# Attention and two mixture layers on one core: two operand loads before two stores, one cast after the exponentials, one pair's values before queries

## The reference

```python
scores = where(block_i >= block_j, q @ k.T / sqrt(64), -1e9)   # blocks of 64
x = softmax(scores) @ v                       # 4 x 8 heads -> (2304, 512)
p = probs / probs.sum(-1)
x = sum(p[:, e] * (relu(x @ w1[e]) @ w2[e]) for e in range(4))  # 512 -> 1024 -> 512
h = x @ w_in                                  # 512 -> 1024
s = h * softmax(h)
out = (layernorm(s) * g_ln) @ w_out           # 1024 -> 512
```

## Time and profile before

| | |
|---|---|
| median of 3 runs | 1154.11 us (1151.96 to 1155.22) |
| the profiled execution | 1155.19 us, span 1153.4 us |
| busy in it: PE, DVE, ACT, POOL | 1136.8, 630.9, 428.1, 418.3 us |
| mean granted PE clock | 0.999 of 2.4 GHz |
| DMA | 146.29 MB, mean 127 GB/s |

### The profile page before, as it was taken

The page is one execution under the profiler, slowest core; times in us unless marked ns, Lnnn a source line. Parts: engine busy times, 40 slices in busy tenths (PEclk is TensorE's granted clock), DMA queues, the critical chain, the costliest instruction groups (busy, mean ns, idle before and its releaser), DMA issues.

```text
span 1153.4 us, 16750 instructions
## 1 busy us (share of the span) xinstructions
PE 1136.8 (99%) x6131; PEld 1021.0 (89%) x6131; DVE 630.9 (55%) x1139; ACT 428.1 (37%) x943; POOL 418.3 (36%) x403
## 2 busy tenths in 40 slices
PE   8999999999999999999999999999999999999998
PEld 8999998879999999999999999999998978888887
DVE  7999887443343524344533334443424478666765
ACT  7998885313223211123221113321112354334432
POOL 8999995645145000024300004400003463432330
PEclk9999999999999999999999999999999999999999
DMA  4766657992825132262304071504025100000000
GB/s 153 230 212 219 227 187 250 364 360 97 306 83 193 43 106 87 83 201 100 147 5 187 1 257 55 218 1 152 40 92 191 48 8 10 29 19 28 19 28 37
DMA packets 68343, 146.29 MB, mean 127 GB/s; under 512 B 6065, under 2 KB 34737, under 8 KB 68273
## 3 DMA queue, kind: packets, MB, share of 16 engines
q1 hardware_dynamic: 68272, 145.36, 36.0%
HBM read 114.60 MB, written 30.74 MB: 126 GB/s over the span
## 4 chain that ended last, share of the span: by engine, by line
PE 79%; POOL 14%; DMA 3%; issue 1%; DVE 1%; ACT 1%; POOLq 0%; SPq 0%; ACTq 0%
PE s L1737 35%; PE outp L1598 19%; PE s L1598 11%; PE ring L1598 10%; DMA x_stash<-x_tmp 2%; POOL qb L703 2%; POOL qb L700 2%; POOL v_hl L713 2%; POOL qb L702 2%; PE ring L1868 1%; DMA q_raw<-in_q 1%; POOL x_tmp L788 1%; POOL v_hl L711 1%; POOL work L764 1%; PE s L1811 1%
## 5 line engine op out<-in xcount | busy, mean ns | idle before, releaser
L1737 PE MATMUL s<-xr,w1s 128*128 128x384 f32 x2016 | 361.1, 337 | 3.3 <-issue 2.2
L1737 PEld LDWEIGHTS s<-xr,w1s 128*128 128x128 f32 x2016 | 351.9, 189 | 8.3 <-issue 2.7
L1075 ACT ACTIVATE hid_h<-u 128x384 fp32r<-128x384 f32 x96 | 50.5, 526 | 372.7 <-DVE u L1423 347.1
L723 POOL TENSOR_TENSOR work<-work 128x256 f32<-128x256 f32 x20 | 14.8, 738 | 393.4 <-DMA work<-in_moe_w 267.5
L1378 DVE SCALAR_TENSOR_TENSOR hid_l<-s,hid_h 128x384 fp32r<-128x384 f32 x48 | 26.7, 557 | 127.0 <-ACT hid_h L1071 127.0
L1737 PE MATMUL s<-w1s,yop_h 128*128 128x512 f32 x252 | 85.7, 399 | 1.9 <-POOL yop_l L878 0.7
L1336 DVE TENSOR_TENSOR u<-s,m_b 128x384 f32<-128x384 f32 x24 | 13.4, 558 | 129.2 <-PE s L1737 129.2
L1071 ACT ACTIVATE hid_h<-s 128x384 fp32r<-128x384 f32 x48 | 23.6, 492 | 155.6 <-PE s L1598 155.6
L1598 PE MATMUL s<-k_h,qb 128*128 128x288 f32 (+8 forms) x320 | 75.8, 324 | 1.6 <-DVE k_l L1232 1.1
L921 ACT ACTIVATE pr<-s,neg_max 128x576 f32<-128x576 f32 (+2 forms) x144 | 75.5, 538 | 1.6 <-DVE neg_max L1220 1.6
L1598 PE MATMUL outp<-w_h,hid_h 128*128 128x512 f32 x192 | 75.5, 393 | 0.0
(11 more groups left out here) (172 smaller groups left out, 2449.2 us busy)
## 6 DMA issues: line engine op xcount, KB each, us to landing
xr<-x_stash SPq DMA_DIRECT2D x77, 768.0 KB, 6.1
r_sb<-r_scratch SPq DMA_DIRECT2D x16, 576.0 KB, 4.2
x_rows<-x_n SPq DMA_DIRECT2D x32, 288.0 KB, 4.5
work<-x_rows SPq DMA_DIRECT2D x24, 384.0 KB, 5.9
x_stash<-x_tmp SPq DMA_DIRECT2D x12, 768.0 KB, 4.4
work<-in_moe_w SPq DMA_DIRECT2D x32, 256.0 KB, 3.8
stage<-in_moe_w SPq DMA_DIRECT2D x32, 256.0 KB, 5.4
x_stash<-xr SPq DMA_DIRECT2D x7, 768.0 KB, 9.3
```

What stands on the lines that cost most here:

```text
L1075: act.activation(hid[slot][0][:, :], source, ACT.Relu).then_inc(hid_high, 1)
L1737: last = pe.matmul(target, x, y, start=start and i == 0, stop=stop and i == 2, skip_group_check=True)
```

## The change

It touches three lists.

On SP, `load_operands` takes a list of names, and the loads of m1's and m2's operands for group 1 are issued in front of `stash_round(1, 1, 2)` and `stash_round(1, 1, 3)`, with the same waits; the other five follow the two rounds as before.

On POOL at p = 13, `split_values(13)` goes in front of `split_query(15)`, with a wait for `v_split` at 14 between them, and the wait for `x_added` at 2 at this point is gone.

On ACT in step 14, the last of the two x casts that stood behind `high(T452)` (round 3 of group 0, second half) goes behind `floor_sums(15)`.

```diff
-            def load_operands(n):
+            def load_operands(n, names=ORDER):
...
-                for name in ORDER:
+                for name in names:
...
             stash_first(range(5, NP))
+            load_operands(1, ("m1", "m2"))
             stash_round(1, 1, 2)
             stash_round(1, 1, 3)
-            load_operands(1)
+            load_operands(1, ("m6", "m7", "m5", "m4", "m3"))
             load_x(2, 1)
...
-                if p in (10, 13):
-                    pool.wait_ge(x_added, 1 + p // 13)
+                if p == 10:
+                    pool.wait_ge(x_added, 1)
...
+                if p == 13:
+                    split_values(p)
+                    pool.wait_ge(v_split, p + 1)
                 if p + 2 < PAIRS:
                     split_query(p + 2)
-                split_values(p)
+                if p != 13:
+                    split_values(p)
...
                 if p == 14:
                     x_cast(0, 1, 2)
-                    x_cast(0, 1, 3)
 
             def late(p):
...
+                if p == 14:
+                    x_cast(0, 1, 3)
```

## The result

The changed kernel takes 1158.64 us (median of 6, 1157.22 to 1159.85); the kernel before, run beside it, 1154.0 us. The ratio is 1.0040 with a 95% interval of 1.0027 to 1.0053: about 4.6 us slower, 3.1 to 6.1 us. The forecast was 1155.2 us, called no change. The profiled execution took 1159.19 us (span 1157.4 us), 4.0 us more than the one of before.

The account below looks back on a forecast made before the run. TensorE, busy for 1136.8 of 1153.4 us, was taken to bound the kernel. Terms of -1.55 - 0.5 + 2.9 + 0.3 = +1.15 us on the median of 1154.11 us gave 1155.2 us, range 1151.5 to 1158.8 us.

Parts of the forecast that it names:

- What bounds the kernel: TensorE, busy every one of 672.1 us from 257.9 us; earlier gains or losses reach the end one for one.
- Values ahead of queries: GpSimd, pair 13's values before pair 15's queries: TensorE's wait on `v_hl` goes, gain 1.55 us, ends 0 and 1.55.
- The cast: ScalarE, last x cast behind the exponentials: TensorE's 1.31 us wait for the reciprocals shrinks, gain 0.5 us, ends 0 and 0.7.
- Loads ahead of stores: SP, start of group 1: round 2's store queues behind two loads, making `m6`'s load 2.9 us later, ends -0.9 and +6.1.
- the signs: Expected in the new profile: no `v_hl` wait, `rinv_wide` wait halved, `m1` without wait, one 5 to 7 us pause before `m6`.
- my upper bound: Round 2's store on SP behind the two loads: at most 7.6 us, landing at 244.9 us.
- The clock: Behind TensorE's pause before `m6`: the same 1.5 us loss as today plus 0.3 us, ends 0 and +1.5.
- The sum: Whole kernel: -1.55 - 0.5 + 2.9 + 0.3 = +1.15 us, counted as no change.
- (a): Rival: round 2's store doesn't queue behind the loads and lands at 240.85 us; 1149.7 to 1151.2 us, chance 0.08.
- (b): Rival: slower by over 0.3%; `m6`'s load takes 7.0 us behind the delayed store, +4.75 us, 1158.9 us, chance 0.16.
- (c): Rival: the attention part, values and cast, gives nothing; +3.2 us, 1157.3 us, chance 0.12.

Follow-up runs that it names:

- e10_down_first_only: The kernel before with only the first two down parts of unit 3 put ahead of m1, m6 and m2 of unit 4: 1150.68 us, ratio 0.9964.
- e7_filled_pause: The changed kernel with 36 matmuls, their result overwritten, between m1 and m6 of unit 4: 1156.65 us, ratio 1.0025 to the kernel before.
- e6_no_stash_wait: The changed kernel with the early loads waiting only for the first three slots' stores: 1156.78 us, ratio 1.0026 to the kernel before.
- e4_values_cast: The kernel before with pair 13's values ahead and the last x cast moved, SP's order as before: 1151.5 us, ratio 0.9972.
- e2_values_only: The kernel before with only pair 13's values ahead of pair 15's queries on GpSimd: 1151.2 us, ratio 0.9977.

## Why the prediction was right and wrong

**What bounds the kernel.** Right. TensorE is busy for all of 668 us from 262 us on; what the change does before that reaches the end whole: the 42 matmuls behind unit 3's down parts start at 261.70 us instead of 257.69 us, 4.0 us later, and the span is 4.0 us longer.

**Values ahead of queries.** Right in its mechanism: the values were ready at 160.3 us (forecast 159.95 us), the 1.55 us wait went, the queries kept 1 us of cover. Measured alone it gave 2.7 us (1.7 to 3.7), more than the wait. A part may be the clock: 9 of its 12 runs had the full clock, against 18 of 29 of the kernel before. The lower clock of the kernel before can stand behind the pauses at unit 4 (its first profile) or behind the very wait on `v_hl` (1.6 us in `e10_down_first_only`). How much of the gain is due to either is argued from these counts, not shown.

**The cast.** The mechanism was right and the size near: 0.41 us off the wait against 0.5 us; in the time it can't be told from nothing. The wait on `rinv_wide` was to be halved, to 0.7 us, and stayed at 0.90 us.

**Loads ahead of stores.** The step, `m6`'s load behind the delayed store, was right in place, in cause and in sign, and mis-sized: the one pause was to be 5.8 us (5 to 7 us among the signs) and was 7.37 us. `m1`'s load was issued when the seventh store landed, as forecast, and took 4.4 us (4.1 us forecast); `m6`'s load took 4.39 us (4.6 us forecast). The failed term is the store of round 2, "3.6 + 2 x 2.0 = 7.6 us less 0.7 us", or 6.9 us. It took 8.38 us, 0.8 us beyond my upper bound. The second load landed at 235.28 + 6.8 = 242.1 us, 2.8 us behind the first and not 2.0 us, and only then the store, 2 us on. With the issue 0.13 us later than forecast, and 1.70 us instead of 2.05 us won in attention (the down parts of unit 2 start at 227.65 us, before at 229.35 us, but at 230.50 us in the second profile of the kernel before), `m6` starts at 248.58 us, 2.72 us later than the 245.86 us of the earlier trace rows, where the sum had +0.85 us: 2.9 less 2.05. Of the difference of 1.9 us, 1.5 (the store) + 0.35 (attention) + 0.13 (issue) - 0.2 (the load) make 1.8 us; the rest is rounding and the gaps between issue and landing.

**The clock.** "I take the same loss again and 0.3 us on top" was wrong, in two ways. Against the profile of before the cost is 1.3 us, not 0.3 us, though still inside the end of 1.5 us: `m6` and `m2` take 4.01 us until the first down part instead of 3.64 us, and the four down parts 9.11 us instead of 8.19 us. The lines of the kernel before and of the changed one, from the down parts' start to that of the products behind them:

```profile
249.50 0.39 PE L1598 MATMUL outp<-w_h,hid_h 128*128 128x512 f32 x1
...
257.69 7.44 PE L1737 MATMUL s<-xr,w1s 128*128 128x384 f32 x42
```

```profile
252.59 0.63 PE L1604 MATMUL outp<-w_h,hid_h 128*128 128x512 f32 x1
...
261.70 7.44 PE L1743 MATMUL s<-xr,w1s 128*128 128x384 f32 x42
```

And against the median the base was wrong: two executions in three of the kernel before have a mean clock of 1.000, so against those the change pays the whole 1.7 to 2.7 us that `e7_filled_pause` gives back. A single profile stood for a kernel that has two outcomes at this place.

In the Trainium skill ("TensorE: Matmul & The Clock Gate", HAM oscillation) a wait of the matmul engine that is long enough brings the lower clock. The traces agree for the long ones: the lower level stands behind the pauses of 7.4 and 7.9 us. It also stands behind one of 2.28 us, and behind 2.16 and 0.55 us, each in one profile, and not behind 0.34 and 0.57 us in another.

**The sum against the trace.** -1.70 + 4.4 + 1.3 = +4.0 us, and 4.0 us lie between the two profiled executions. The forecast had -2.05 + 2.9 + 0.3 = +1.15 us. That the median still fell into the range is partly luck: it stands 0.16 us inside, and the forecast itself was 3.4 us short. The call of no change was wrong: the loss of 4.6 us is over the 3.5 us that it wanted, a case to which the prediction gave 0.19.

**The rivals.** (a), the store that doesn't queue, is refuted by `e6_no_stash_wait` against `e4_values_cast`: the queue ahead costs 4.4 us. (b) gave the time, 1158.9 against 1158.64 us, with its threshold of 5.5 us passed by 4.4 + 1.3 us, but its split was wrong: it put the delay in `m6`'s load (7.0 us), which took 4.39 us; the delay was in the store. (c) is refuted by `e2_values_only` and `e4_values_cast`. The argument that I held against (b), fewer transfers in the queue, was right for the load and said nothing of the store.

## What to carry to other kernels

In this kernel a transfer moved ahead of another on SP's queue was paid for twice: the other was issued late by the wait that the first carries (3.2 us), and landed later by the bytes of the first (4.4 us). Before moving it, ask which of the two feeds the consumer that comes next; here the load that was early (`m2`) was third in line and the store that was late fed the second. Where a few microseconds of other ready work stand right behind a late operand, put a part of them in front of it, and keep the rest for what comes late next.

## What the runs showed of the hardware

A pause of 2.2 + 0.5 us of TensorE had the lower clock behind it in one execution and pauses of 0.3 + 0.6 us had not in another of the same program; behind a wait of 2.28 us, elsewhere in the same program but for two down parts (`e10_down_first_only`), it was down again. The mean granted clock split the 76 timed runs of the kernel before 51 to 25, with medians 1.2 to 3.65 us apart. A profile of one execution doesn't show that executions differ; the clocks of the timed runs do, though not where the clock fell.

The 768 KB load of `m1` took 7.4 us from issue to landing with two stores issued just ahead of it and 4.4 us behind an empty queue. The store of 768 KB took 4.9 us with no load ahead of it and stores of group 0 still in the queue, and 9.5 us with these and two loads; with group 0's stores landed it took 6.8 us behind one load and 8.4 us behind two.
